# Attention with two scans per step: the prefix scan put first, two products and two evictions of the second pass swapped, and GpSimd's inversions held back

## What is computed

```python
for t in range(S):
    y[:, :, t] = np.einsum('bhd,bhde->bhe', rt, state)
    Sa = np.einsum('bhde,bhe->bhd', state, at)
    state_decay = state * wt[:, :, None, :] - np.einsum('bhd,bhe->bhde', Sa, bt)
    state = state_decay + np.einsum('bhd,bhe->bhde', vt, kt)
```

## Time and profile before

| | us |
|---|---|
| median of 3 runs (lowest, highest) | 1057.15 (1055.74, 1058.28) |
| the profiled execution's own time | 1054.7 |
| its span, first to last instruction | 1052.9 |
| first pass (first scan to first g2) | 5.4 to 134 |
| second pass | 134 to 373 |
| routing, then the two expert stages | 373 on |
| busy: TensorE, VectorE, ScalarE, GpSimd | 952.9, 711.5, 442.8, 268.6 |
| mean granted clock of TensorE | 0.982 |

### The profile page before, as it was taken

How to read it: one execution, slowest core, us unless ns; L and a number is a source line. 1 busy time by engine, 2 the same in 40 slices (tenths; PEclk the granted TensorE clock), 3 DMA queues, 4 the chain that set the end, 5 groups by cost and what they waited for, 6 DMA issues and landing times. The chain is left out here.

```text
span 1052.9 us, 48691 instructions
## 1 busy us (share of the span) xinstructions
PE 952.9 (90%) x21425; PEld 874.8 (83%) x21425; DVE 711.5 (68%) x1076; ACT 442.8 (42%) x940; POOL 268.6 (26%) x348
## 2 busy tenths in 40 slices
PE   3526779999999998999999999879999999999997
PEld 2426769999999958998999999668999999999997
DVE  8997958899988764555555555567666565656664
ACT  5525635755555604545555555513222212222211
POOL 1009989798900003222111100241001000000000
PEclk9999988999999999999999999999999999999999
DMA  7968866898898539998676755120100101010100
GB/s 220 234 173 189 203 140 188 242 246 236 238 243 241 150 119 307 332 294 278 190 249 214 228 169 169 41 79 13 38 1 26 26 1 26 2 26 1 26 1 26
DMA packets 116866, 153.19 MB, mean 145 GB/s; under 512 B 68516, under 2 KB 87860, under 8 KB 116420
## 3 DMA queue, kind: packets, MB, share of 16 engines
q1 hardware_dynamic: 102468, 118.68, 40.3%
q0 software_dynamic: 5872, 25.28, 7.8%
q10 hardware_dynamic: 8464, 8.43, 2.4%
HBM read 126.72 MB, written 19.23 MB: 139 GB/s over the span
## 5 line engine op out<-in xcount | busy, mean ns | idle before, releaser
L1468 ACT CAST g_hi<-g 128x512 fp32r<-128x512 f32 x96 | 59.5, 620 | 278.0 <-DVE g L1412 274.4
L1321 PE MATMUL y_bank<-w_out_hi,g_hi 128*128 128x320 f32 x380 | 119.0, 313 | 5.1 <-DVE g_lo L1386 4.3
L1109 PE MATMUL h_bank<-xt,w 128*128 128x128 f32 x992 | 122.0, 282 | 1.8 <-issue 1.8
L1149 DVE TENSOR_TENSOR w_lo<-w_all,w_hi 128x640 fp32r<-128x640 f32 x124 | 101.7, 826 | 31.9 <-ACT w_hi L1189 27.0
L1109 PEld LDWEIGHTS h_bank<-xt,w 128*128 128x128 f32 x992 | 115.8, 195 | 6.0 <-issue 2.2
L1321 PE MATMUL y_bank<-w_out_hi,g_lo 128*128 128x320 f32 x380 | 118.0, 310 | 0.0
L1321 PE MATMUL y_bank<-w_out_lo,g_hi 128*128 128x320 f32 x380 | 117.9, 310 | 0.0
L1408 DVE TENSOR_SCALAR neg<-h_bank,slope 128x512 f32<-128x512 f32 x96 | 72.0, 750 | 65.8 <-PE h_bank L1308 65.4
L1308 PE MATMUL h_bank<-xt_hi,w_in_hi 128*128 128x512 f32 x288 | 113.1, 393 | 0.5 <-DVE xt_hi L1369 0.5
L1308 PE MATMUL h_bank<-xt_hi,w_in_lo 128*128 128x512 f32 x288 | 112.1, 389 | 0.0
L1386 DVE TENSOR_TENSOR g_lo<-g,g_hi 128x512 fp32r<-128x512 f32 x96 | 66.5, 693 | 65.9 <-ACT g_hi L1468 64.5
(11 more groups left out here) (213 smaller groups left out, 2145.1 us busy)
## 6 DMA issues: line engine op xcount, KB each, us to landing
w<-w_in SPq DMA_DIRECT2D x31, 1024.0 KB
t_in<-wak_in SPq DMA_DIRECT2D x24, 679.0 KB, 5.7
t_in<-wab_in SPq DMA_DIRECT2D x21, 679.0 KB, 5.0
w_all<-w_in POOLq DMA_DIRECT2D x8, 1280.0 KB, 9.2
rr<-rr_in SPq DMA_DIRECT2D x24, 336.0 KB, 3.5
w_rest<-w_in SPq DMA_DIRECT2D x62, 128.0 KB
vtm<-vtm_in SPq DMA_DIRECT2D x24, 240.0 KB, 3.7
vt<-vt_in SPq DMA_DIRECT2D x24, 224.0 KB, 4.0
```

Source lines behind the costliest of these rows:

```text
L1109: last = pe.matmul(h_bank[s][h][:, f * ET:(f + 1) * ET], w1[s][:, k, (FH * h + f) * PARTS:(FH * h + f + 1) * PARTS], xt[s][:, k, :], start ...
L1149: dve.tensor_tensor(piece(w2_lo, p), of_expert(e, p), piece(w2_hi, p).bitcast(F32), ALU.subtract).then_inc(s_w2lo, 1)
L1321: last = pe.matmul(y_bank[n][:, 0:FEAT], g_part[j % RING][:, n * PARTS:(n + 1) * PARTS], v[:, f, :], start=f == 0 and p == 0, stop=f == NF ...
L1468: act.copy(g_hi[j % RING][:, :], g[j % 2][:, :]).then_inc(s_ghi, 1)
```

## The change

Three things change. (1) The prefix scan comes first in every step, the reciprocal of its column C starts the suffix scan; the small copy of the chunk's whole product into wq's last column goes (that product is wq's column C already), `alpha` comes ahead of `second`, and what waited for alpha (t_in's loads on SP, g1 on TensorE) waits for `second`. `cross_wq` waits for a later y. (2) In the second pass TensorE runs sat ahead of sa and m2 ahead of the state's last product; ScalarE and VectorE evict in that order. (3) POOL's first inversion waits for `second` of step `POOL_AT` = 15 + 8 // 2 = 19 of the first pass.

```diff
+POOL_AT = AT_JOIN + JOINED // 2
...
                 if j >= TR:
-                    if j - TR < STEPS:
-                        sp.wait_ge(s_alpha1, j - TR + 1)
-                    elif j - TR == STEPS:
-                        sp.wait_ge(s_alpha0, 1)
-                    else:
-                        sp.wait_ge(s_second, j - TR + 1)
+                    sp.wait_ge(s_second, j - TR + 1)
...
             def cross_wq(k):
-                sp.wait_ge(s_wc, k + 1)
-                if k >= 3:
-                    sp.wait_ge(out_of["y"], k - 1)
+                sp.wait_ge(s_wq, STEPS + k + 1)
+                if k >= 2:
+                    sp.wait_ge(out_of["y"], k)
...
             for k in range(STEPS):
+                prefixes(k)
+                suffix_starts(k)
                 suffixes(k)
-                prefix_starts(k)
-                prefixes(k)
                 if k >= 1:
                     dve.wait_ge(did["bt"], k)
+                scaled_alpha(k)
                 scaled_second(k)
-                scaled_alpha(k, s_alpha1)
...
                 if more:
-                    scaled_alpha(STEPS + k + 1, s_alpha)
+                    scaled_alpha(STEPS + k + 1).then_inc(s_alpha, 1)
                 if k + 2 < STEPS:
-                    suffixes(STEPS + k + 2)
+                    if k >= 1:
+                        dve.wait_ge(out_of["y"], k + 1)
+                    prefixes(STEPS + k + 2)
...
                 if k + 2 < STEPS:
-                    prefixes(STEPS + k + 2)
+                    suffixes(STEPS + k + 2)
...
+                dve.wait_ge(did["m2"], k + 1)
+                masked(m2, BA).then_inc(out_of["m2"], 1)
                 dve.wait_ge(did["st"], k + 1)
...
                 last.then_inc(out_of["st"], 1)
-                dve.wait_ge(did["m2"], k + 1)
-                masked(m2, BA).then_inc(out_of["m2"], 1)
...
+            pool.wait_ge(s_second, POOL_AT + 1)
             for n, g in enumerate(BY_POOL):
...
+                act.wait_ge(did["sat"], k + 1)
+                act.copy(by_row(sat[:, :, :]), wide(BA)).then_inc(out_of["sat"], 1)
                 act.wait_ge(did["sa"], k + 1)
                 act.copy(flat(sa_tm[:, :, :]), narrow(BC)).then_inc(out_of["sa"], 1)
-                act.wait_ge(did["sat"], k + 1)
-                act.copy(by_row(sat[:, :, :]), wide(BA)).then_inc(out_of["sat"], 1)
...
+                heads(sat_product, BA, C, done="sat")
                 heads(sa_product, BC, DIM, done="sa")
-                heads(sat_product, BA, C, done="sat")
                 heads(from_s(lambda i, q, m: at_m(rr, i, q, m, live(m))), BB, C, opens=False, closes=False)
+                arrive(out_of["sat"], i)
+                heads(m2_product, BA, C, done="m2")
                 arrive(out_of["sa"], i)
                 heads(from_b(lambda i, q, m: sa_tm[rows(m), slot(q ^ m, i), :]), BD, DIM, opens=False, done="st")
-                arrive(out_of["sat"], i)
-                heads(m2_product, BA, C, done="m2")
```

More of the change, by code:

```diff
@@ L237, in attention @@
         s_step, s_step_dve = m_.sem("s_step"), m_.sem("s_step_dve")
-        s_set, s_suf, s_rw, s_wq, s_wc, s_second, s_alpha1, s_alpha0, s_alpha = (m_.sem(n) for n in (
-            "s_set", "s_suf", "s_rw", "s_wq", "s_wc", "s_second", "s_alpha1", "s_alpha0", "s_alpha"))
+        s_set, s_suf, s_rw, s_wq, s_second, s_alpha0, s_alpha = (m_.sem(n) for n in (
+            "s_set", "s_suf", "s_rw", "s_wq", "s_second", "s_alpha0", "s_alpha"))
         names = ("turned", "across", "joint", "g1", "bt", "w", "s", "u", "ktm", "z", "m1", "sa", "sat", "st", "g2", "m2", "y", "pick")
@@ L431, in own_and_crossed, with prefixes, suffix_starts @@
                 return wq_both[(STEPS + k) % 3][:, :, part].rearrange("q (g p) t -> q g p t", p=HP)[:, 0:3:2]
+            def prefixes(j):
+                dve.wait_ge(s_t[j % TR], 16 * (j // TR + 1))
+                if j >= 1:
+                    dve.wait_ge(s_suf, j)
+                dve.tensor_tensor_scan(out=forward(wq[j % 3][:, :, :]), data0=forward(w_of(j)), data1=forward(restart[:, :, :]), initial=0.0,
+                                       op0=ALU.mult, op1=ALU.add).then_inc(s_wq, 1)
+            def suffix_starts(j):
+                dve.wait_ge(s_wq, j + 1)
+                dve.reciprocal(restart[:, :, WIDE - 1:WIDE], wq[j % 3][:, :, C:C + 1]).then_inc(s_rw, 1)
             def suffixes(j):
-                dve.wait_ge(s_t[j % TR], 16 * (j // TR + 1))
+                dve.wait_ge(s_rw, j + 1)
                 if j >= 2:
@@ L438, in suffixes, with scaled_second, scaled_alpha @@
                                        op0=ALU.mult, op1=ALU.add).then_inc(s_suf, 1)
-            def prefix_starts(j):
+            def scaled_second(j):
                 dve.wait_ge(s_suf, j + 1)
[L442 to L452, removed]
                 dve.tensor_tensor(second[:, :, :], in_of(j, 1), suf[j % 2][:, :, 2:WIDE], ALU.mult).then_inc(s_second, 1)
-            def scaled_alpha(j, sem):
-                dve.tensor_tensor(alpha[:, :, :], in_of(j, 0), wq[j % 3][:, :, 0:C], ALU.mult).then_inc(sem, 1)
+            def scaled_alpha(j):
+                return dve.tensor_tensor(alpha[:, :, :], in_of(j, 0), wq[j % 3][:, :, 0:C], ALU.mult)
             def y_out(k):
@@ L548, in _ @@
                 else:
-                    dve.wait_ge(s_wqx[(k + 1) % 2], 32 * turn(k + 1))
+                    dve.wait_ge(s_wqx[k % 2], 32 * turn(k))
                     last = dve.tensor_tensor(by_row(swt), BD[:, :, 0:HP * DIM].rearrange("q r (p e) -> q r p e", e=DIM),
-                                             own_and_crossed(k + 1, slice(WIDE - 1, WIDE)).to_broadcast([PARTS, 2, HP, DIM]), ALU.mult)
+                                             own_and_crossed(k, slice(C, C + 1)).to_broadcast([PARTS, 2, HP, DIM]), ALU.mult)
                 last.then_inc(out_of["st"], 1)
-                dve.wait_ge(did["m2"], k + 1)
-                masked(m2, BA).then_inc(out_of["m2"], 1)
                 if more:
@@ L927, in _ @@
             warm(2)
-            pe.wait_ge(s_alpha0, 1)
+            pe.wait_ge(s_second, STEPS + 1)
             heads(with_alpha(second), BC, C, done="g2")
```

18 lines of the change are left out of this document (9 added, 9 removed).

## The result

The changed kernel takes 1068.31 us (median of 7 executions, 1061.19 to 1077.07), beside 1055.74 (1053.39 to 1058.28) for the kernel before in as many: the ratio is 1.0119, with a 95% interval of 1.0077 to 1.0161. So it is slower by some 12.6 us, where +4.9 was predicted.

A forecast was written before the change was run, and what follows sets the result against it. VectorE was taken to bound the first pass, TensorE the second. Terms -2.3 + 0.4 + 7.6 - 0.8 = +4.9 us on the profiled 1054.7 gave 1059.6; that execution lying 2.4 below the median, the forecast was 1062.0, range 1053 to 1066.

The forecast's parts named there:

- Part 1: POOL's later start in the first pass: 2.3 us less, and 0.4 more for second-pass steps under POOL.
- Part 2: The scans' new order, dropped copy and later waits: worth nothing, the copy's time being idle anyway without POOL.
- Hidden, with about 2 us to spare. vtm's load keeps its time.: On SP, t_in's load goes out 1.3 us later behind cross_wq but is needed a step later; vtm's load is unmoved.
- fourth rival: SP is blocked too, by POOL's end past 322, vtm's turn or the shifted t_in load: 4 more, 1066; 12%.
- Part 3: Second-pass reordering: picks wait 0.6 us for the state's eviction, 0.41 a step, 0.3 under POOL; 7.6 more, less 0.8.
- The 0.8 for absorbed transfers: In the second pass, longer steps give DMAs more time, as a few start late for vtm and rr: 0.8 less.
- The 0.23 for "faster": Chance of the whole kernel being faster by over 0.2%: the first rival's 14% and most of the second rival's 10%.
- second rival: No new wait at the picks: vtm and ax set the steps' starts and absorb TensorE's 0.4; 1055.3; 10%.
- First rival: Where the passes meet, TensorE's gap shortens below some 2.5 us and the clock may not fall: 9 less, 1053; 14%.
- GpSimd beside VectorE: By the skill's port lock, first-pass steps under POOL would take 8 us, the last four costing 14 more; not adopted.

The follow-up runs named there:

- e2: Kernel before with only POOL's first inversion held back to step 19 of the first pass: 1057.21 us, ratio 1.0011.
- e4: Changed kernel, with SP's cross_wq waiting for a state's eviction in place of y's: 1061.63 us, ratio 1.0056 to the kernel before.
- e6: Kernel before with the new scan order, cross_wq waiting for the state's eviction, old GpSimd start, old product order: 1045.79 us, ratio 0.9943.
- e14: e6 repeated unchanged on another chip: 1048.91 us, ratio 0.9968 to the kernel before.
- e12: e6 with GpSimd's wait count set to 11, which moved nothing, so in effect e6 again: 1052.33 us, ratio 0.9988 to the kernel before.
- e17: Changed kernel with only the t_in load issued ahead of cross_wq on SP: 1060.96 us, ratio 1.0061 to the kernel before.
- e1: Kernel before with only the second pass's reordering (sat ahead of sa, m2 ahead of the state's product, evictions likewise): 1063.95 us, ratio 1.0099.
- e3: Changed kernel with the second pass's reordering undone on TensorE, ScalarE and VectorE: 1059.57 us, ratio 1.0033 to the kernel before.
- e7: e6 with GpSimd's inversions starting from step 19: 1050.53 us, ratio 0.9988 to the kernel before.
- e19: e7 repeated unchanged: 1054.82 us, ratio 0.9985 to the kernel before.
- e8: Kernel before with only sat's product and copy ahead of sa's, m2 left in place: 1059.72 us, ratio 1.0067.
- e5: Kernel before with the new scan order and cross_wq waiting for yt as in the change, nothing else: 1060.32 us, ratio 1.0072.
- e16: e6 with the t_in load issued ahead of cross_wq on SP: 1054.15 us, ratio 0.9985 to the kernel before.
- e10: e1 with y's product moved ahead of the picks, and yt's eviction waiting for the picks: 1051.99 us, ratio 1.0012 to the kernel before.
- e15: e5 with the t_in load issued ahead of cross_wq on SP: 1055.03 us, ratio 0.9997 to the kernel before.
- e18: e6 with GpSimd's inversions starting from step 17: 1049.91 us, ratio 0.9953 to the kernel before.

## Why the prediction was wrong, point by point

- **Part 1** (-2.3, +0.4). Its steps came true: GpSimd starts at 104.92, steps 19 to 23 save 2.2 of the 2.9 us, e2 alone starts the second pass 2.1 us earlier. GpSimd ends at 305.9 in the change and at 311 to 316 in e2 to e4. But no timing shows a gain; the term, taken as a gain in the end, was some 2 to 5 us too good.
- **Part 2** ("nothing"). Wrong twice, here and in the next point. The scans' order shortens a step of the first pass by 0.13 us while VectorE is its bound, because an instruction no longer waits for the scan just ahead of it: e6, e14 and e12 give -3.5 us on average. I had counted operations and a copy, and not the wait on the first pass's bound engine.
- **"Hidden, with about 2 us to spare. vtm's load keeps its time."** This is the step that failed. The shift of t_in was sized well (1.24 us against yt, 1.35 against the step, 1.3 forecast), and vtm is still issued when z allows. What I asked was when t_in is needed, not what its 679 KB run beside: vtm and ax land 1.1 and 1.5 us later. I put this at nothing; e4 and e17 price it at 6.6 and 6.1 us. The fourth rival had this shift in it, at 4 us and 12%; its price was near and its chance too low.
- **Part 3** (+7.6 - 0.8). The mechanism, to a few hundredths of a microsecond at five places, as forecast. The size: 10.4 us alone (e1), 9.1 and 7.3 in the change (beside e3; e4 beside e7 and e19). Missing were 0.1 a step at the loop's start, and the steps under GpSimd, where 0.3 was taken and e1 has 0.45. The 0.8 for absorbed transfers is borne out: the kernel before has 0.8 us of waits for vtm in its second pass, e1 none. I split off the picks' wait rightly but didn't see that half of the swap alone costs as well (e8).
- **The sum.** The measured kernels give a path on which each difference is one term: the scans' order -3.5 us (e6, e14, e12), GpSimd's late start on it +2.1 (e7, e19; some 3 either side), the swap on both +7.3 (e4), the late load on all +6.6 (the change). That is 12.5, beside 12.6 measured; forecast were 0, -1.9, +6.8 and 0. So the late load is the largest miss, GpSimd's start the second, and the scans' order hid a part of both. The range ended at 1066, the fourth rival's own price; it had left out that rival's worst, which is near what came.
- **The chances.** The 0.23 for "faster" counted most of the second rival, whose own 1055.3 lies 0.17% under the median, inside the 0.2% called no change. This doesn't touch the forecast.
- **First rival.** Fallen: in the change the gap is 3.83 us (3.55 before) and the clock stays low longer. Nor does the gap's length decide, as I had it: it is 2.45 us in e5 and 3.56 in e16, and the granted clock from 140 to 175 us is 0.66 and 0.90 (0.71 before, 0.54 in the change). In both profiles the gap is the place where the queue that the page calls "q8 instruction" carries one block (from 139.3 to 143.0 in the change, from 142.4 to 145.9 before), and once the loop is on its way it carries none (155 to 390, 160 to 370). That fits TensorE waiting for code in the first round of a new loop. If so, this trace again speaks against the Trainium skill (Runtime: NRT & Kernel Launch, on instruction fetch), by which prefetch hides it.
- **GpSimd beside VectorE.** The first-pass steps 19 to 23 take 4.7 us with GpSimd started, far from the 8 us that the prediction worked out from the Trainium skill (SBUF — State Buffer, on port contention). What fails is that working, not the page. Rows of VectorE and GpSimd, first pass of the kernel before:

```profile
102.07 1.68 DVE L437 TENSOR_TENSOR_SCAN suf<-t_in,restart 128x528 f32<-128x528 f32 x1
102.72 1.50 POOL L127 TENSOR_TENSOR solved<-solved,share 128x252 f32<-128x252 f32 x1
...
104.03 1.31 DVE L446 TENSOR_TENSOR_SCAN wq<-t_in,restart 128x528 f32<-128x528 f32 x1
104.30 1.48 POOL L124 TENSOR_TENSOR share<-solved,blk 128x255 f32<-128x255 f32 x1
```

GpSimd's instruction ends 0.47 and 0.44 us behind the scan. So it is in the whole trace with the 34 of its large ones (240 elements or more to a partition) that start beside a scan, `alpha` or `second`: they take 0.95 to 1.56 us and end 0.40 to 0.59 behind that instruction, where 28 that run beside nothing of VectorE's take 0.61 to 0.73. Each waits for the other in turn, as the page says; but a wait is only what is left of the other's instruction, under half a microsecond for the scan (1.69 for 1.25), and not the 1 us each that the prediction took.

## What to carry to other kernels

Before a semaphore on a DMA-issuing queue is exchanged for a later one, look at the largest transfer behind it, and ask whose small transfers it will run beside: a load that is itself in time can make others late. If a product is moved ahead to have its result earlier, move its consumer too (e10), or the engine stands with the result in hand. And when parts of a change are priced by profiles, time each one alone as well: one part's 2 us at a stage's end was not found in the kernel's time, and a wait that I had not counted was worth some 3.5.

## What the hardware showed that I had not expected

A short stand of TensorE can cost more than itself. Behind waits of 1.28 us (the change, step 6), 2.46 (e5, step 13), 2.15 (e15, step 6) and 1.51 us (e16, step 6) the groups go at nearly double their time, for up to two steps: such a step takes 13 to 14 us instead of 9 to 9.5. The granted clock between 212 and 236 us is 0.62 in the change and 1.00 in the kernel before. Waits of 1.52 us for vtm in e18 (step 8) and 1.20 in e3 (step 14) left it full, and one of 0.91 in e12 (step 14) did not, so the length alone doesn't decide. Where the passes meet it is the same: from 140 to 175 us the granted clock is 0.90 in the profiles of e7, e12, e16, e17 and e18, and 0.54 in that of the change. I take this for a cause of the spread within one kernel: over its 12 executions e6 has clocks of 0.979 to 0.990, and the two lowest are those of its two slowest executions.

The granted clock in the profile is not all there is to TensorE's pace. The first rival took it that gaps in the first pass "left the clock full"; it reads 1.00 there, but g1's products take 1.13 us in every step, and the same product in the second pass takes 0.69 at a granted clock of 1.00 and 1.11 at half. Why, no run here shows.

The spread itself is larger than I had allowed. The kernel before has 1044.91 to 1062.74 us over the chips, and three kernels that do the same (e6, e14, e12) came out at 0.9943, 0.9968 and 0.9988 of it, with intervals of 0.0025 to 0.003 either side. Differences of 0.3% between kernels of different chips are not told apart here.
